# A fused attention and two-layer MoE kernel on one core: five buffer areas moved 352 bytes down in the partition

## The reference

```python
qn = q / (norm(q, axis=1) + 1e-6); kn = k / (norm(k, axis=1) + 1e-6)   # norms over the tokens
a = softmax(kn.T @ qn / tau)                 # 256 x 256
x = v @ a                                    # N x 256
h = x @ w_in                                 # N x 2048
g = where(h >= 1, h, where(h <= -1, 0, (h + 1)**2 / 4))
y = g @ w_out                                # N x 256
xn = y / sqrt(mean(y*y) + 1e-6) * rms_g
gate = xn @ w_gate; val = xn @ w_val         # N x 1536
out = (gate * sigmoid(gate) * val) @ w_out2  # N x 256
```

## Time and profile before

| | |
|---|---|
| three runs | 1147.46, 1148.35 and 1150.86 us, median 1148.35 |
| the profiled execution | 1147.29 us |
| its span, first to last instruction | 1145.5 us |
| busy PE, PEld | 1126.5 us (98%), 949.7 us (83%) |
| busy DVE, ACT, POOL | 862.3 us (75%), 802.8 us (70%), 1.0 us |
| mean granted TensorE clock | 0.998 |
| DMA | 48.86 MB, mean 43 GB/s |

### The profile page before, as it was taken

One profiled execution on the slowest core, in us unless ns is written; L12 is line 12 of the kernel. 1 busy time (PEld: TensorE's weight loads), 2 busy tenths in 40 slices (PEclk: granted clock), 3 DMA queues, 4 the chain that ended last, 5 costly groups with the idle time before them and its releaser, 6 DMA issues.

```text
span 1145.5 us, 15766 instructions
## 1 busy us (share of the span) xinstructions
PE 1126.5 (98%) x5708; PEld 949.7 (83%) x5708; DVE 862.3 (75%) x1257; ACT 802.8 (70%) x1160; POOL 1.0 (0%) x9
## 2 busy tenths in 40 slices
PE   8999999999999999999989999999999999999998
PEld 7857778878878878888878888888888888888997
DVE  5768887877877887889878877776777767666555
ACT  5668898898898898888866565567557456456544
POOL 0000000000000000000000000000000000000000
PEclk9999999999999999999999999999999999999999
DMA  9800112002012010022140011011002001000100
GB/s 345 293 15 1 22 35 55 1 36 39 1 38 32 1 38 0 1 78 64 54 132 1 1 56 38 1 32 60 17 1 74 1 1 62 9 1 1 38 1 33
DMA packets 72064, 48.86 MB, mean 43 GB/s; under 512 B 43186, under 2 KB 62258, under 8 KB 71986
## 3 DMA queue, kind: packets, MB, share of 16 engines
q1 hardware_dynamic: 71986, 47.85, 13.8%
HBM read 35.52 MB, written 12.32 MB: 42 GB/s over the span
## 4 chain that ended last, share of the span: by engine, by line
PE 92%; DVE 3%; ACT 2%; issue 1%; DMA 1%; SPq 0%; DVEq 0%; ACTq 0%
PE ps L1185 17%; PE ps L1186 16%; PE ps L1187 16%; PE ps L1203 8%; PE ps L1205 7%; PE ps L1204 7%; PE ps L1229 6%; PE ps L1233 5%; PE ps L1231 5%; PE ps L1244 3%; DMA qk_sb<-in_k_dram 1%; DVE cg L772 1%; ACT out_sb L419 1%; DVE cv L772 0%; PE ps L1155 0%
## 5 line engine op out<-in xcount | busy, mean ns | idle before, releaser
L419 ACT ACTIVATE s<-ps 128x512 f32<-128x512 f32 (+1 forms) x360 | 209.9, 587 | 44.5 <-PE ps L1187 29.4
L1185 PE MATMUL ps<-xc_hi,wc_hi 128*128 128x512 f32 (+1 forms) x504 | 202.7, 402 | 8.5 <-ACT s L419 4.4
L1186 PE MATMUL ps<-xc_lo,wc_hi 128*128 128x512 f32 (+1 forms) x504 | 198.1, 393 | 0.0
L1187 PE MATMUL ps<-xc_hi,wc_lo 128*128 128x512 f32 (+1 forms) x504 | 196.3, 389 | 0.0
L1229 PE MATMUL ps<-wo_hi,h_hi 128*128 128x256 f32 x564 | 159.2, 282 | 0.0
L1231 PE MATMUL ps<-wo_lo,h_hi 128*128 128x256 f32 x564 | 158.9, 282 | 0.0
L1233 PE MATMUL ps<-wo_hi,h_lo 128*128 128x256 f32 x564 | 158.6, 281 | 0.0
L419 ACT ACTIVATE h_hi<-cg 128x512 fp32r<-128x512 f32 (+1 forms) x144 | 89.0, 618 | 93.0 <-DVE cg L878 89.5
L1203 PE MATMUL ps<-g_hi,wo_hi 128*128 128x512 f32 (+1 forms) x384 | 150.8, 393 | 0.4 <-DVE g_lo L788 0.2
L1204 PE MATMUL ps<-g_lo,wo_hi 128*128 128x512 f32 (+1 forms) x384 | 149.2, 389 | 0.0
L1205 PE MATMUL ps<-g_hi,wo_lo 128*128 128x512 f32 (+1 forms) x384 | 149.1, 388 | 0.0
(11 more groups left out here) (124 smaller groups left out, 1920.4 us busy)
## 6 DMA issues: line engine op xcount, KB each, us to landing
out_dram<-out_sb SPq DMA_DIRECT2D x11, 512.0 KB, 2.9
qk_sb<-in_q_dram SPq DMA_DIRECT2D x10, 512.0 KB, 10.2
qk_sb<-in_k_dram SPq DMA_DIRECT2D x10, 512.0 KB, 10.6
y_scratch<-y_sb SPq DMA_DIRECT2D x10, 512.0 KB, 3.0
xraw<-y_scratch SPq DMA_DIRECT2D x10, 512.0 KB, 4.6
vstage<-in_v_dram SPq DMA_DIRECT2D x64, 64.0 KB, 2.4
wo_raw<-in_moe_w_out_dram SPq DMA_DIRECT2D x7, 512.0 KB, 9.6
w_in_raw<-in_moe_w_in_dram SPq DMA_DIRECT2D x4, 512.0 KB, 12.1
```

Source lines behind the costliest of these rows:

```text
L419: return nc.scalar.activation(dst, src, ACT.Copy, **kw)
L1185: nc.tensor.matmul(dst, w_h, x_h, start=p in ("p1", "p2", "p7"), stop=False, skip_group_check=True)
L1186: nc.tensor.matmul(dst, w_h, x_l, start=False, stop=False, skip_group_check=True)
L1187: nc.tensor.matmul(dst, w_l, x_h, start=False, stop=True, skip_group_check=True).then_inc(made[p], 1)
```

## The change

Two lines change. The areas XC, XR, GA, O1 and O2 move down by 352 bytes, onto the end of the tables at IV (offset M + 118272), and the arena that reserves the space becomes 320 bytes smaller. No instruction, operand size, order or semaphore changes.

```diff
-        arena = ctx.enter_context(nc.sbuf_tensor("arena", [P, 53200], F32))
+        arena = ctx.enter_context(nc.sbuf_tensor("arena", [P, 53120], F32))
         BASE = 16512
...
         M = 2048
         W, H, Q, S = M, M + 57344, M + 73728, M + 81920
         VS, YA, RA, XS, IV = M + 88064, M + 96256, M + 100352, M + 108544, M + 116736
-        XC, XR, GA, O1, O2 = M + 118624, M + 147296, M + 161632, M + 178016, M + 194400
+        XC, XR, GA, O1, O2 = M + 118272, M + 146944, M + 161280, M + 177664, M + 194048
```

## The result

The changed kernel takes 1136.8 us (median of 4 runs, 1136.2 to 1138.0) against 1147.9 before: ratio 0.9902, 95% interval 0.9879 to 0.9925. The profiles show one execution each, of 1147.3 us before and 1138.0 us changed.

The account below looks back on a forecast made before the run. PE's own matmul pace was taken as the bound. First products -2.0 us, with pieces, DVE, ACT and DMA at 0, gave 1146.4 us against the median 1148.35, called no difference; range 1141.3 to 1152.0.

Parts of the forecast that it names:

- The bound: Whole kernel: PE's own matmul pace sets the time, busy 98% of 1145.5 us.
- DVE and ACT at zero: Instructions on moved buffers: at most 1 ns each, 2.4 us of work off the path, counted as 0.
- DMA at zero: Transfers into moved areas such as xraw: any change in their length is hidden, counted as 0.
- The 4%: Transfers into moved areas: 4% shorter by the skill's beat count for rows of 2048 bytes, hidden.
- The 120 ns step of the last pieces: 256-column matmuls near the end: step expected still at 120 ns if the forecast holds.
- first products: Matmuls reading xc as moving data: 2376 gain 0.83 ns each, 2.0 us less, sized from aligned xs trios.
- my upper reading of 6.3: First products by shown mean lengths: 792 trios gain 8 ns each, 6.3 us less.
- Pieces: Matmuls with both operands in moved areas: distance unchanged, so 0; at 0.83 ns each, 2.4 us less.
- rival B: First products: operands equally far from a multiple of 64 go better together; 6.3 us less, 1142.1; chance 0.19.
- A: All fp32r matmuls: alignment sets their pace, 218 ns for 512 columns; 69 us less, 1079; chance 0.03.
- C: Aligned trios in succession: only the third matmul's loss remains; 4.7 us more, 1153.0; chance 0.10.
- D: Partition's base not where BASE puts it: buffers swap distances, no difference; counted with the forecast, together 0.68.

Follow-up runs that it names:

- experiment 10: PE alone, ones as data, rest left out, in the kernel's own order and places for each layout: 10.457/10.440 us a group before (even/odd), 10.213/10.200 changed.
- experiment 8: Changed kernel with every area from W to O2 32 bytes higher: 1137.6 us, ratio to before 0.9908.
- experiment 11: Changed kernel with all five areas 128 bytes higher, still at multiples of 64: 1145.0 us, ratio to before 0.9971.
- Experiment 12: PE alone, ones as data, weights and data places taking turns, then second-layer groups: 226.5 ns a matmul all in phase, 233.3 with weights always 32 apart.
- experiment 3: Changed kernel with GA (g, h) 32 bytes past a multiple of 64, O1 and O2 64 higher: 1139.3 us, ratio to before 0.9918.
- experiments 2: Changed kernel with XR (xraw) 32 bytes past a multiple of 64, GA, O1 and O2 64 higher: 1139.2 us, ratio to before 0.9917.
- experiment 7: Changed kernel with XC 32 bytes past a multiple of 64, areas behind it 128 higher: 1147.5 us, ratio to before 0.9998.
- experiment 13: Changed kernel with h_hi and h_lo at GA + 64, O1 and O2 256 higher: 1134.5 us, ratio to before 0.9878.
- experiment 14: Changed kernel with h_hi and h_lo at GA + 192, O1 and O2 256 higher: 1134.6 us, ratio to before 0.9883.
- experiment 15: Changed kernel unaltered, on the same chip as the two with h moved: 1137.1 us, ratio to before 0.9898.
- experiments 1: Changed kernel with XC 32 bytes past a multiple of 64, the other four areas 64 higher: 1145.9 us, ratio to before 0.9973.
- experiment 4: Changed kernel with O1 and O2 (output weights) 32 bytes past a multiple of 64: 1141.6 us, ratio to before 0.9936.
- experiment 5: Changed kernel with all five areas 64 bytes higher: 1137.2 us, ratio to before 0.9908.
- experiment 6: Changed kernel with XR 32 bytes past a multiple of 64, areas behind it 128 higher: 1138.9 us, ratio to before 0.9925.

## Why the prediction was wrong

**What was right.** The bound: PE's own pace and 98% of the span. DVE and ACT at zero: durations equal to 1 ns, busy times within 1.6 us. DMA at zero: landing of the transfers to `xraw` was 4.0/4.5/7.1 us and is 4.0/4.6/6.8, and PE waits for none of them. The 4% that the prediction worked out from the Trainium skill, DMA: Bandwidth & Descriptors, section How a descriptor splits into AXI transactions, is not seen; that section speaks of bytes that are fetched, and the moved side here is the one that is written. PE's idle time before line 1185 stayed: 4.6 us for ACT and 2.9 for DVE's line 772 before, 4.9 and 3.0 changed. The 120 ns step of the last pieces stayed too.

**The step that failed** is the comparison that sized the first products: "This is just what the change makes of all the others." I took `xs` trios before, aligned, with aligned weights, as a sample of the aligned kernel and found 0.83 ns a matmul. The sample's own place was right, but a matmul's step also depends on the places that PE reads in the matmuls around it, and those were still 96 bytes off modulo 256. Two trios in a row don't get free of it: in phase everywhere, the same `xs` trios take 0.68 us instead of 0.69, and PE alone with the layout of before gives 10.440 us for the odd group, the real one's time exactly (experiment 10). The term was put at 2.0 us. With the steps from start to start of all matmuls of these lines added up, it was 591.6 us before and is 582.9: 8.7 us less, above even my upper reading of 6.3.

The sample was also read from an unlucky stretch. Of the four even groups, the first took 10.415 us and the other three 10.453, while all odd ones took 10.44. The three steady groups alone differ by 0.04 us over 18 matmuls, 2.2 ns each, and the same sum would have given 5.3 us.

**Pieces, taken at nothing.** My reason was that weights and data share their distance before and after. The same neglect: they stand between product trios that don't. In the steady groups of tile 2 a piece's trio went from 0.695 to 0.680 us and a product's from 0.699 to 0.680. Over the kernel, the 512- and 448-column pieces gained 2.7 us, and the 256-column ones lost 0.5. My range ended at 1141.3, from rival B's 6.3 us and the scatter of the runs; the 2.4 us that I named for the pieces was not added to it. The result is 4.5 us below that end.

**The total.** 8.7 + 2.7 - 0.5 = 10.9 us, within 0.2 the 7.3 + 3.8 = 11.1 us by which the two layers became shorter. In the first layer, tiles 1 to 4 gave 1.6 or 1.7 each and tile 0, where PE waits, 0.6. Tile 5 with 448 columns gave 0.1: what the 512-column matmuls gain, those with 448 don't, and I had counted 372 of them with the rest. In the second layer a group of tile 3 gained only 0.07 us against 0.24 in the first layer's tile 2: its trios p1, p2, p7 and p6 went from 0.70 to 0.68 or 0.69, and p4 and p5, which stand between 256-column pieces, stayed at 0.70.

**The rivals.** B, "moving data and weights with the same distance from a multiple of 64 go better together", was right in kind and had a chance of 0.19. It was sized by the same sample of `xs`, 6.3 us against 11.1, and held to be weak because four groups with `xs` were only 20 ns shorter. Its modulus is 256 and not 64, and by its own rule the pieces would have gained nothing. A was wrong in size and in what it says of absolute alignment: the step of 226.7 ns that remains is far from 218, and experiments 8 and 11 exclude alignment as such. C fell: the third matmul of an `xs` trio went down to 389 ns. D, that the base isn't where it seems, would have been harmless, but not for the reason that I gave: experiment 8 moved everything by 32 bytes and nothing changed, so only the distances between the areas count.

The Trainium skill, TensorE: Matmul & The Clock Gate, section Step-by-step: what each phase is for, says that PE has two independent read ports and that loading the next weights takes no read bandwidth from the running matmul. If that were all, the place of the weights would not matter. Experiment 12 measures 226.5 and 233.3 ns for the same matmuls with only that place changed, so the measurement decides: some dependence between the reads is there. The Trainium skill, SBUF — State Buffer, section Specifications (TRN2), gives lines of 16 bytes. All places here, before and after, are multiples of 32, so no operand begins inside such a line in either kernel.

**What stays open** is which reads meet: weights of the next matmul with the data of this one, own weights with own data, or one matmul's end with the next one's beginning. Experiment 12 shows that none of the first two alone explains the steps, and that both together don't either (231.1 ns expected, 234.7 measured with only the weights taking turns). Also open is why 64 apart costs 2.5 ns and 128 apart 6.6, and why 512-column matmuls are fastest in phase while the 256-column ones are not.

## What to carry to other kernels

Where a kernel is bound by dense fp32r matmuls with 512 moving columns and new weights for each, try all buffers that PE reads at the same distance modulo 256 bytes; their absolute alignment to 64 was worth nothing by itself. It was 3% of such a matmul's step. With 448 columns the kernel gained nothing, and 256-column matmuls were faster out of phase, so a mix needs its own table of places. And don't take a few instructions that already have the property as a sample of a kernel that has it throughout: vary it in a run of its own, with PE alone, where a table of places costs one run.

## What the runs showed of the hardware that I hadn't expected

- The distance modulo 256 as above, 512 columns and PE alone: 226.7 ns in phase, 229.2 at 64, 233.3 and more at every other multiple of 32 up to 224.
- In the second layer's mix of 512 and 256 columns the best place found is not in phase: h 64 bytes apart gives 7.57 us a group and in phase 7.67 with PE alone, and 7.71 against 7.75 in the real kernel. The gain is in the 256-column matmuls: down to 113 ns from about 120.
- After the same wait the clock falls for a stretch in some profiles and not in others. PE waits 2.2 us for ACT at the start of the second layer in all of them. Windows behind that wait in the changed kernel, then in experiment 3 (us; PE, PEld, DVE, ACT, POOL; clock, DMA share, GB/s):

```profile
585.50:589.00 3.50, 3.46 (x11) 3.07 (x12) 2.57 (x4) 2.77 (x5) 0.00 (x0) 0.51 0.49 159
```

```profile
590.60:594.00 3.40, 3.38 (x22) 3.12 (x23) 3.40 (x6) 3.03 (x5) 0.00 (x0) 1.00 0.46 147
```

  Behind it, the first runs at 0.51 of the full clock, that is at 1.2 GHz, and gets 11 matmuls done in 3.5 us, the second stays at 2.4 GHz and gets 22 done in 3.4. The group takes 11.77 us or 10.22. The kernel before fell too, and so did experiments 2, 7, 8 and 13 to 15; experiments 1, 3, 4, 5, 6 and 11 didn't. It can differ between executions of one kernel: the four of experiment 5 had a mean granted clock of 1.000 twice and of 0.998 twice. So 1.5 us of a comparison of single profiles here may be the clock, more than some layouts differ by.
- In the changed kernel's profile another fall, in the window from 51.2 to 56 us (0.69 on average), goes with the later start of the first layer, 69.4 against 67.6 us: PE's instructions were 0.13 us late at 50.6 and 1.76 at 57.2. In the profile of the same kernel unaltered (experiment 15) that window ran at the full clock and the first layer still began at 69.4, this time late from the start: PE had waited 1.05 us for a load of k at 25 us, and was 1.8 us late from 30 us on.
